# A chain of linear attention, routed experts and a dense layer on one core: the order of the first gathers, the products with a zero state, and filler products

## What is computed

```
k_n = k / (norm(k) + 1e-06)
state = zeros(B, H, D, D)
for t in range(S):
    y[t] = q[t] @ state
    v_old = k_n[t] @ state
    state = state + beta[t] * outer(k_n[t], v[t] - v_old)
```

## Time and profile before

| what | value |
|---|---|
| median of 3 timed runs | 1024.1 us |
| lowest and highest of them | 1023.5 and 1026.5 us |
| the profiled execution | 1020.8 us |
| its span (first to last instruction) | 1019.1 us |
| its mean granted TensorE clock | 0.979 |
| attention block | 0 to 337.7 us |
| routing for the first expert, to the first expert product | 337.7 to 372.6 us |
| experts and dense layer | 372.6 to 1019.1 us |

### The profile page before, as it was taken

How to read it: one execution, slowest core, us unless ns; L and a number is a source line. 1 busy time by engine, 2 the same in 40 slices (tenths; PEclk the granted TensorE clock), 3 DMA queues, 4 the chain that set the end, 5 groups by cost and what they waited for, 6 DMA issues and landing times.

```text
span 1019.1 us, 32577 instructions
## 1 busy us (share of the span) xinstructions
PE 949.1 (93%) x14016; PEld 886.2 (87%) x14016; DVE 641.2 (63%) x1563; ACT 417.0 (41%) x962; POOL 525.3 (52%) x653
## 2 busy tenths in 40 slices
PE   4899899898988589999999999999999999999997
PEld 3788788887777469999999999999999999999997
DVE  6877677776665587777767657757657758632000
ACT  3445444444443044263353344344335335326322
POOL 3235555555560056285376467458448449438533
PEclk9899999999999679999999999999999999999999
DMA  9322222211110040210300300220030040030000
GB/s 311 122 66 67 66 67 66 59 51 51 51 43 20 9 147 1 101 48 24 119 30 24 124 24 24 73 75 24 18 131 24 1 140 24 9 132 24 16 1 24
DMA packets 34767, 61.97 MB, mean 61 GB/s; under 512 B 3904, under 2 KB 23488, under 8 KB 34240
## 3 DMA queue, kind: packets, MB, share of 16 engines
q1 hardware_dynamic: 31552, 50.45, 15.3%
q0 software_dynamic: 3072, 9.44, 2.8%
HBM read 50.44 MB, written 9.44 MB: 59 GB/s over the span
## 4 chain that ended last, share of the span: by engine, by line
PE 62%; DVE 2%; POOL 2%; DMA 0%; issue 0%; ACT 0%; POOLq 0%; DVEq 0%
PE PS L1503 59%; POOL xgT L1139 1%; PE PS L1482 1%; PE PS L1469 1%; PE PS L1521 1%; DMA xg<-x_rows,idx 0%; POOL act_t L1139 0%; PE PS L1454 0%; POOL w_lo L1143 0%; DVE over L1319 0%; PE PS L1488 0%; DVE hits L1330 0%; POOLq L1004 0%; DVE cand L1348 0%; DVE delta L1338 0%
## 5 line engine op out<-in xcount | busy, mean ns | idle before, releaser
L1139 POOL TENSOR_TENSOR act_t<-whole,act_t 128x384 fp32r<-128x384 f32 x192 | 198.7, 1037 | 251.4 <-ACT whole L1212 250.5
L1206 ACT ACTIVATE act_t<-PS 128x384 fp32r<-128x384 f32 x192 | 94.4, 492 | 350.4 <-PE PS L1503 350.4
L1503 PE MATMUL PS<-w_out_hi,act_t 128*128 128x384 f32 x768 | 222.8, 345 | 0.5 <-POOL act_t L1139 0.5
L1503 PE MATMUL PS<-x2T,w_in_hi 128*128 128x384 f32 x768 | 219.1, 342 | 0.0
L1503 PEld LDWEIGHTS PS<-x2T,w_in_hi 128*128 128x128 f32 x768 | 141.4, 188 | 0.8 <-ACT x2T L1204 0.4
L1503 PEld LDWEIGHTS PS<-w_out_hi,act_t 128*128 128x128 f32 x768 | 139.7, 188 | 1.0 <-POOL act_t L1139 0.8
L1503 PE MATMUL PS<-w_out_lo,act_t 128*128 128x384 f32 x384 | 130.8, 341 | 0.0
L1503 PE MATMUL PS<-x2T,w_in_lo 128*128 128x384 f32 x384 | 130.7, 340 | 0.0
L1503 PE MATMUL PS<-xgT,w_hi 128*128 128x384 f32 x384 | 108.4, 341 | 2.3 <-POOL xgT L1139 1.7
L1503 PE MATMUL PS<-act_t,w_hi 128*128 128x384 f32 x384 | 105.7, 335 | 0.0
L1143 POOL TENSOR_TENSOR w_lo<-w_sb,w_hi 128x384 fp32r<-128x384 f32 x64 | 69.6, 1102 | 52.5 <-ACT w_hi L1217 52.5
(11 more groups left out here) (231 smaller groups left out, 1824.0 us busy)
## 6 DMA issues: line engine op xcount, KB each, us to landing
w_sb<-moe_w SPq DMA_DIRECT2D x16, 768.0 KB, 5.3
w_sb<-moe_w SPq DMA_DIRECT2D x8, 1536.0 KB, 10.1
k_in<-k_t SPq DMA_DIRECT2D x24, 192.0 KB, 3.1
KQ<-q_t SPq DMA_DIRECT2D x48, 96.0 KB, 2.2
v_in<-v_t SPq DMA_DIRECT2D x24, 192.0 KB, 2.6
x_rows<-ysb SPq DMA_DIRECT2D x48, 96.0 KB, 2.2
w_in<-moe_w_in SPq DMA_DIRECT2D x1, 3072.0 KB, 12.7
w_out<-moe_w_out SPq DMA_DIRECT2D x1, 3072.0 KB, 21.0
```

The lines of the kernel that those rows point to most:

```text
L1139: nc.gpsimd.tensor_tensor(lo, whole_of(t), hi.bitcast(F32), ALU.subtract).then_inc(rest_ok, 1)
L1206: nc.scalar.activation(hi, src, func).then_inc(hi_ok, 1)
L1503: ins = mm(o, a, b, start=start, stop=stop, skip_group_check=True)
```

## The change

Five things are done.

1. The head. GpSimd sets ones16 first of all; TensorE multiplies it with itself (`fill`, 128x128 by 512 columns, into a bank that nobody reads) 18 times before its first wait, and 3, 5, 3, 3 and 3 times at the places below. ScalarE takes L1T of tile 0 around take_k(1) rather than after square(4).
2. No products with the zero state: from_state and read_state start with tile 2, the first two right sides and B are copies of vs, the first two states are copies of PSUM, and the semaphores that counted these products are waited for with numbers lower by two (loads of q and copies of k for tiles 3 and 4 wait for GP_ps).
3. The end of the block: SyncE's wait for the stores of x_rows goes to GpSimd, ahead of the first gather. The second of the last two copies of logits is made by VectorE.
4. The indices: the differences of the thirds are taken in tok3, behind the first piece of hot, and not after the placing; two instructions take another form (a tensor_tensor with a broadcast for a tensor_scalar).
5. GpSimd's order for the first expert: the three gathers ahead of the rests of w1.

```
-            for b in range(2):
-                nc.gpsimd.memset(St[b][0][:, :, :], 0.0).then_inc(zero_ok, 1)
+            nc.gpsimd.memset(rc["ones16"][:, :], 1.0).then_inc(ones_ok, 1)
...
             root(1, 1, 4)
             take_k(0)
+            take_l1t(0, 0)
             take_k(1)
+            take_l1t(0, 1)
             square(4)
-            for g in range(G):
-                take_l1t(0, g)
...
-                if j == 0:
-                    dve.wait_ge(KS_ps, n + 1)
+                if j == 0 and n < 2:
+                    dve.wait_ge(vs_ok, n + 1)
+                    nc.vector.tensor_copy(rb[:, :], vs[n][:, :]).then_inc(rb_sb, 1)
+                elif j == 0:
+                    dve.wait_ge(KS_ps, n - 1)
...
+            def fill(times):
+                for _ in range(times):
+                    mm(PS[:, 5, :], rc["ones16"][:, :], rc["ones16"][:, :].unsqueeze(1).to_broadcast([C, 4, C]),
+                       start=True, stop=True, skip_group_check=True)
+
+            pe.wait_ge(ones_ok, 1)
+            fill(18)
             pe.wait_ge(mask_ok, 8)
+            pe.wait_ge(zero_ok, 4)
             turn_k(0)
+            fill(3)
             products(0)
             turn_k(1)
+            fill(5)
             level2(0)
+            fill(3)
             level4(0)
+            fill(3)
             level8(0)
...
-                from_state(n)
+                if n >= 2:
+                    from_state(n)
...
                 prod24(n)
+                if n == 0:
+                    fill(3)
...
-                read_state(n)
+                if n >= 2:
+                    read_state(n)
...
             sp.wait_ge(w_ld, 32)
-            for p in range(2):
-                sp.wait_ge(y_st[p], 32 * NT // 2)
...
-            for q in range(2):
-                split_w1(0, q)
+            for p in range(2):
+                pool.wait_ge(y_st[p], 32 * NT // 2)
             for j in range(MT_TOK):
                 gather(0, j)
-            split_w1(0, 2)
+            for q in range(3):
+                split_w1(0, q)
...
+                    if h == 0:
+                        chain(v.tensor_tensor(tok3[:, :, 0:4:3, :], tok[:, :, :].unsqueeze(2).to_broadcast([C, NT, 2, 2]),
+                                              past[:, :, :].unsqueeze(3).to_broadcast([C, NT, 2, 2]), ALU.mult))
+                        v.tensor_tensor(tok3[:, :, 1:3, :], tok3[:, :, 3:7:3, :], tok3[:, :, 0:4:3, :], ALU.subtract).then_inc(tok_ok, 1)
...
-                v.tensor_copy(idx_f[:, MT_TOK - 1, :], placed[:, MT_TOK - 1, :]).then_inc(dv, 1)
-                chained["n"] += 1
-                chain(v.tensor_copy(idx_s[:, :, :], placed))
-                chain(v.tensor_tensor(idx_f[:, 0:MT_TOK - 1, :], idx_s[:, 0:MT_TOK - 1, :], idx_s[:, 1:MT_TOK, :], ALU.subtract))
+                chain(v.tensor_copy(idx_s[:, :], placed[:, :, 1]))
...
-                v.scalar_tensor_tensor(idx[r % 2][:, :], idx_f[:, :, 0], float(C), idx_f[:, :, 1], ALU.mult, ALU.add).then_inc(idx_ok, 1)
+                v.scalar_tensor_tensor(idx[r % 2][:, :], placed[:, :, 0], float(C), idx_s[:, :], ALU.mult, ALU.add).then_inc(idx_ok, 1)
...
                     pe.wait_ge(hot_ok, NT // HOT * r + h + 1)
+                    if h == 0:
+                        pe.wait_ge(tok_ok, r + 1)
```

More of the change, by code:

```diff
@@ L45, in busy, with attention @@
         nc.tensor.matmul(PS[:, bank, 0:DM], w[:, 0, 0:C], w[:, 0, :], start=True, stop=True, skip_group_check=True)
-def attention(nc, k_t, v_t, q_t, beta_t, wg, x_rows, logits, identf, up_f, rc, PS, wi, wo, w_in, w_in_hi, w_in_lo, w_out, w_out_hi, w_out_lo):
+def attention(nc, k_t, v_t, q_t, beta_t, wg, x_rows, logits, identf, up_f, rc, PS, ysb, y_st, wi, wo, w_in, w_in_hi, w_in_lo, w_out, w_out_hi, w_out_lo):
     ctx = ExitStack()
@@ L356, in take_logits @@
                 c = n // 2
-                for b in range(2):
+                for b in range(2 if n < NT - 1 else 1):
                     m = (2 * (n % 2) + b) * (S // C) + c // 2
@@ L656, in _ @@
                 take_s(n)
+            dve.wait_ge(lg_ps, NT)
+            c = (NT - 1) // 2
+            nc.vector.tensor_copy(logits[CH * (c % 2):CH * (c % 2) + CH, NT - 1, :], PS[rows(1), 7, DM:DM + E]).then_inc(lg_sb, 1)
         @block.tensor
@@ L758, in correct @@
                         pe.wait_ge(Y_sb, n)
-                if j == 2:
-                    pe.wait_ge(QS_ps, n + 1)
+                if j == 2 and n >= 2:
+                    pe.wait_ge(QS_ps, n - 1)
                 for i in range(HG):
@@ L772, in apply @@
                     pe.wait_ge(H_ok, n + 1)
+                if j == 0 and n == 1:
+                    pe.wait_ge(S_sb, 1)
                 each(lambda h, b: mm(PS[rows(b), 6, col(h)], Hm[n % 2][rows(b), h, :], X[n % 2][rows(b), col(h)],
@@ L988, in fill_routing_constants @@
     n += 1
-    for t in ("onesrow", "ones16", "ones_b"):
+    for t in ("onesrow", "ones_b"):
         nc.gpsimd.memset(k[t][:, :], 1.0).then_inc(filled, 1)
@@ L995, in fill_routing_constants, with experts @@
     nc.gpsimd.tensor_copy(k["tok"][:, :, :], k["tok_i"][:, :, :]).then_inc(shaped, 1)
-    nc.gpsimd.tensor_copy(k["tok3"][:, :, 0, :], k["tok_i"][:, :, :]).then_inc(shaped, 1)
+    nc.gpsimd.tensor_copy(k["tok3"][:, :, 6, :], k["tok_i"][:, :, :]).then_inc(shaped, 1)
     nc.gpsimd.tensor_copy(k["tri16"][:, :], up_f[:, :]).then_inc(shaped, 1)
-def experts(nc, x_rows, w1, w2, w_in_hi, w_in_lo, w_out_hi, w_out_lo, out, logits, identf, up_f, rc, PS):
+def experts(nc, x_rows, w1, w2, w_in_hi, w_in_lo, w_out_hi, w_out_lo, out, logits, identf, up_f, rc, PS, y_st):
     ctx = ExitStack()
@@ L1656, in program @@
         rc = routing_constants(sb)
+        ysb = [sb(f"ysb{p}", [C, DM]) for p in range(2)]
+        y_st = [ctx.enter_context(nc.semaphore(f"y_st{p}")) for p in range(2)]
         PS = ctx.enter_context(nc.psum_tensor("PS", [C, 8, 512], F32))
-        attention(nc, k_t, v_t, q_t, beta_t, wg, x_rows, logits, identf, up_f, rc, PS, wi, wo, w_in, w_in_hi, w_in_lo, w_out, w_out_hi, w_out_lo)
-        experts(nc, x_rows, w1, w2, w_in_hi, w_in_lo, w_out_hi, w_out_lo, out, logits, identf, up_f, rc, PS)
+        attention(nc, k_t, v_t, q_t, beta_t, wg, x_rows, logits, identf, up_f, rc, PS, ysb, y_st, wi, wo, w_in, w_in_hi, w_in_lo, w_out, w_out_hi, w_out_lo)
+        experts(nc, x_rows, w1, w2, w_in_hi, w_in_lo, w_out_hi, w_out_lo, out, logits, identf, up_f, rc, PS, y_st)
 def kernel(**inputs):
```

56 lines of the change are left out of this document (28 added, 28 removed).

## The result

| what | before | after |
|---|---|---|
| median of ten timed runs each, on one chip | 1027.14 us | 1014.66 us |
| lowest and highest | 1023.5 and 1034.8 us | 1013.0 and 1020.8 us |
| the profiled execution, and its span | 1020.8, 1019.1 us | 1016.6, 1014.8 us |
| attention block ends at | 337.7 us | 338.1 us |
| first expert product | 372.6 us | 372.1 us |

The ratio is 0.9872, with a 95% interval from 0.9851 to 0.9893: 12.5 us faster by the medians, where 1.7 us were forecast. The profiled execution of before was shorter than all ten of its timed runs, so the two profiled executions differ by 4.2 us only. They lay the difference where the forecast didn't look: at the first expert product the kernels are 0.5 us apart, and the remaining 3.8 us lie behind it.

A forecast was written before the change was run, and what follows sets the result against it. TensorE, busy 93% of the span, was taken as the bound, with gains only in its waits before 373 us. Head and zero state 1.0, block's end 0.5, gathers 0.2: 1.7 us off 1024.1 gives 1022.4 us, range 1019.5 to 1025.2 us.

The forecast's parts named there:

- The v_in bound: Tile 1: level4's second half can't start before 34.97 us, behind v_in's load; 1.25 us of 4 to 6 us survive.
- head and zero state: Fillings and dropped zero-state products up to prod24(1): together 1.0 us, bounds -0.3 and 2.6 us.
- The zero state: Tiles 0 and 1: four groups of 32 products at 0.68 us go; counted with the head in 1.0 us.
- The end of the block: Attention block's end: store wait moved 0.33 us, logits' copies split 0.14 us; together 0.5 us.
- The gathers: Before the first expert product: gathers ahead of w1's rests gain 0.2 us, bounds -0.3 and 0.7 us.
- ScalarE's rounding of w2 would be last: Before the first expert product: xgT's copy waits for ScalarE's w2 rounding, so at most 0.7 of 1.45 us arrive.
- The digit search and tok3 at nothing: Routing: changed forms and reordering gain 0.3 us, tok3's two differences cost 0.3 us; nothing in sum.
- From 373 us on nothing in the diff touches that stage's matmuls: Expert stage: its matmuls are untouched, so everything has to come from the first 373 us.
- The difference on the profiled execution: Whole kernel: 1.7 us off the profiled 1020.8 us, carried to the three timed runs' median, 1024.1 us.
- (B): Rival: clock stays at 2.4 GHz over the wait for v_in; 3.3 to 3.8 us gained, 1020.6 us; chance 0.25.
- (C): Rival: slower, clock falls in the v_in wait and doesn't return in tile 1; 1028.0 us if back at 53 us; 0.10.
- I take it that the clock falls in it: TensorE's 3.5 to 5 us wait before 35 us: clock falls there, comes back 3 to 7 us after 35 us.

The follow-up runs named there:

- before_v2: The kernel before with only SyncE's load of v_in for tile 2 issued ahead of w_out's 3 MB; ratio 0.9997.
- lay_before: The kernel before with 3424 unused bytes a partition ahead of the expert stage's tensors, placing them as in the changed kernel, first run; ratio 1.0000.
- lay_again: The kernel before with the same 3424 unused bytes ahead of the expert stage's tensors, second run; ratio 0.9979.
- route: The kernel before with the change's parts from the attention block's end on: store wait, logits split, tok3 and indices, gathers first, and their placing; ratio 0.9946.
- after_aligned: The changed kernel with 32 more unused bytes ahead of the expert stage's weights, addresses again on multiples of 64; ratio 0.9894 to before.
- splits_first: The changed kernel with two rests of w1 again ahead of the three gathers on GpSimd; ratio 0.9884 to before.
- head_zero: The kernel before with the head's fillings and without the products with the zero state; routing, block's end and placing as before; ratio 0.9958.
- head_zero_lay: The kernel before with the head's fillings, no zero-state products, and 3424 unused bytes ahead of the expert stage's tensors; ratio 0.995.
- after_third: The changed kernel, unchanged, timed a third time against before, on another chip; ratio 0.9921.
- before_again: The kernel before, unchanged, as a second kernel against itself; 1028.76 us, ratio 0.9998.

## Why the prediction was wrong

The stages, as means over traces (us; "low" is time at 1.2 GHz). The four traces of before include before_v2, which has the earlier load of v_in. The old attention code is in these four, lay_before, lay_again and route. The new one is in the changed kernel's four, after_aligned, splits_first, head_zero and head_zero_lay.

| stage | old attention code, 7 traces | head and zero changed, 8 traces |
|---|---|---|
| to B of tile 2 | 56.9 (55.7 to 58.3) | 55.0 (53.4 to 56.4) |
| from there to the block's end | 288.9 (281.9 to 295.7) | 285.5 (281.7 to 293.0) |
| low in the latter | 11.8 | 9.4 |

| stage | before, 4 traces | the changed kernel, 4 traces |
|---|---|---|
| estar to first expert product | 15.9 to 17.6 | 15.6 to 16.4 |
| first turn | 82.8, all four | 82.5 (84.1 with 4 us low) |
| from there to the end | 563.67, all four | 560.1 to 560.2 |

Point by point:
- **The v_in bound held in the first pair, by luck of the trace.** The half of level4(1) came at 35.99 us after a wait of 3.09 us (forecast 35.0 us, 3.5 us or more), and the full clock came back at 44 us, where 38 to 42 us were taken. But in the other three traces of the changed kernel the wait is 0.8 us once and nothing twice: with the clock low from 24 or 25 us on, TensorE itself came there only at 34.7 us. The size was off too: by the means 1.9 us of head and zero state are left at tile 2 instead of 1.0 us (1.7 us without before_v2). The forecast stood on one trace of before whose B of tile 2 was among the earliest of seven: 55.8 us, mean 56.9 us.
- **The zero state** was forecast as a part of 1.0 us behind the head. Alone it gave 0.9949, so most of its gain doesn't need the head. How four groups of 0.68 us give 4 to 5 us at the end isn't settled. The attention block behind tile 2 was 3.4 us shorter with head and zero state changed, but its length spreads by 4 us (one standard deviation) in either column, so this is no proof; 0.5 us of it is the end of the block in those kernels that have it. Over all twenty traces that length follows two things (a least-squares fit, which leaves 6% of the variation): 0.35 us for each us of low clock, and 1.1 us for each us of TensorE's "issue" stops, 15.7 to 23.0 us a trace. The columns differ by 2.4 us in the first and 1.0 us in the second, so 1.9 of the 3.4 us go with these two, and no run ties either to an edit.
- **The end of the block**: 0.5 us forecast, 0.8 us measured (1.27 us became 0.49 or 0.50 us in every trace that has the edit). The mechanism was right. The block's own exchange was not the 0.6 us that "stays": 0.33 us are left behind the last copy.
- **The gathers**: forecast 0.2 us with 0.7 us as the bound. From estar to the first expert product the changed kernel's four traces have 16.0 us on average and those of before 16.5 us: 0.5 us, with a spread of 0.8 and 1.6 us. The step that failed is that ScalarE's rounding of w2 would be last: in the earlier trace rows already xgT waited 0.71 us more, for TensorE, and it waited for TensorE in all twenty traces. The gathers a microsecond earlier didn't slow the load of w2: from its issue to ScalarE's start it took 10.1 us in after, 10.0 us in splits_first, 10.8 us before. In after xgT then waited 0.75 us for TensorE, and TensorE for the first gather. The page of the Trainium skill that was cited for gathers and loads sharing engines, "DMA: Bandwidth & Descriptors" (Issuing engines are not separate DMA queues), isn't contradicted; in all these kernels the gathers are issued inside the load, and a difference by their order couldn't be seen.
- **The digit search and tok3 at nothing**, "in later rounds this lies beside expert products": this step failed. That work lies beside expert products, but TensorE takes its counts from there, and in the first turn the meeting of one tiny VectorE instruction with GpSimd's run decides 1.9 us. In the search for the first expert, from the block's start to estar, the change gave 0.1 us (18.58 us became 18.44 us).
- **"From 373 us on nothing in the diff touches that stage's matmuls"**: false in effect, and the step that failed most. The diff moves their operands, and the forecast put this at nothing: 3.8 us from the first expert product on, the largest single term. 3.5 us of it lie in the seven later turns and are shown by the placing alone; 0.3 us lie in the first, which placing alone makes longer. The sizes in tok3 and the allocation of ysb were in the diff.
- **The difference on the profiled execution.** It took one short run as the measure; three timed runs gave 1024.1 us as before's median, ten gave 1027.1 us, and 112 further ones in the other sittings 1029.8 us.
- **Rivals.** None of them held it: (B), the fastest, was 6 us too slow. (C) has its mechanism in the traces: after_third's clock is low for 27 us in all behind tile 2, and that trace is the longest of the changed kernel; but before has low stretches there as well, 3.5 to 13.7 us in three traces and 23.9 us in before_v2.
- **The clock around the wait.** "I take it that the clock falls in it" is a step that failed: TensorE waited from 32.90 us, and the granted clock was 0.50 from 30.3 to 43.9 us. From 24.0 us to that fall TensorE was busy 3.7 of 6.3 us, with a stop of 1.50 us. The rule of the Trainium skill ("TensorE: Matmul & The Clock Gate", HAM oscillation) that a pause puts the engine back on the half clock can't be tested on this wait, since the clock was low when it began.

Added up from traces: 3.8 us from the first expert product on, 1.9 us to tile 2, 0.8 us the block's end, 0.5 us gathers and indices, 0.1 us digits, and 2.9 us (3.4 less 0.5) in the attention block that stay unproven: 10.0 us of the 12 us that four timings give.

## What to carry to other kernels

Before calling a stage untouched, list which tensors the diff moves, and then read one turn's length in both traces to the hundredth: here it was the most exact number in a trace, the same to 0.01 us in four traces of before. Tiny VectorE instructions that a TensorE count waits for should be looked up against GpSimd's long runs, at every place where a shift of a microsecond can bring them together. And one profiled execution is a sample: here two traces of one kernel differ by 7 us, more than most edits are worth, so an edit's small terms need the stage's spread over several traces. A wait and a low clock in one place don't show which came first: compare the start of each, and look for a trace that has only one of them.

## What the runs showed of the hardware

- The same 128x128 by 384 products, with the stationary piece of act_t at another place in SBUF, took 342 instead of 345 ns from start to modelled end (768 products with w_out_hi, before against lay_again), and followed one another after 181 instead of 184 ns. The whole turn was 0.5 us shorter. The addresses were 3424 bytes higher (turns of 79.42 us) or 3456 bytes higher (79.36 us). The runs show that the place matters, not by what rule; w1, w2, xgT, x2T, act_t and osb moved together, and none was tried alone.
- A VectorE instruction of three elements took 0.17 us in most places, and 0.76, 0.84 or 2.85 us in the second expert's search, where GpSimd ran operations back to back. There it ended 24 to 39 ns behind the end of a GpSimd operation in all twenty traces.
- In the attention block the granted clock fell to 1.2 GHz in stretches of 3.4 to 13.7 us, 0 to 27.3 us in all behind tile 2, while TensorE was about nine tenths busy with small products (254.9 of 287.7 us in before_again). There the block was about 0.39 us longer for each microsecond at the low level (slope over twenty traces), close to the 0.43 us of the forecast. In the 112 further timed runs of before a whole run was 0.22 us longer for each microsecond, routing included.
- 18 multiplications of ones took 6.68 us, the first 13 starting 0.43 us apart and the last five 0.21 us apart, and the record has the full clock from 6.4 us. It was low again from 13.2 us for 3.4 us.
- With such fillings the clock was low for 10.2 to 20.5 us between 21 and 45 us in eleven of twelve traces, without them for 0 to 6.8 us in eight. What the fillings have to do with it is not shown beyond this count.
